# First expert's weights in quarters behind each head's copies, and rough scores and scores issued earlier

## The chip, the cores and the metric

The kernel runs on one NeuronCore of a Trainium2 chip. The metric is the device time of one execution in microseconds (us). All times below come from timed runs or from one profiled execution of the same program.

## The reference

Three stages follow each other, in float32. Attention has 2 batches, 8 heads, 576 positions and head size 64, with a causal mask and a bias from a running sum of `s`. Its output, 1152 rows of 512, goes through a sparse mixture of 8 experts (two experts a row), and then through a second mixture in which every row visits all 8 experts.

```python
scores = scale * q @ k.T                      # attention, per batch and head
scores = where(causal, -1e9, scores + minimum(-(cum_i - cum_j), 0))
attn = exp(scores - max); attn /= attn.sum(-1) + 1e-9
x = (attn @ v)                                # 1152 x 512
...
h = maximum(x[mask] @ w1[e], 0)               # sparse: the two best experts of a row
out[mask] += top2_w * (h @ w2[e])
...
out += P[:, e:e+1] * (maximum(x @ w1[e], 0) @ w2[e])   # dense: all 8 experts, P balanced in 8 steps
```

## The kernel before

Each engine runs its own written-out list of instructions, and they meet at semaphores. The change touches the attention stage and its borders only.

Attention is cut into 80 steps `k`: 8 heads, two halves (batches) a head, five tiles a half. Five steps are a unit, ten are a head. In step `k` TensorE (PE) issues, in this order: the rough scores of a later step (`rough`, L567), which exist only to find each row's maximum; transposes that turn the row maxima into a row (`turn_max`, L579), at two places in a unit; the scores of a later step (`scores`, L598 and L599); and the product of the probabilities with v (`mix`, L614). VectorE (DVE) takes each row maximum (L1041). ScalarE (ACT) puts turned maxima in place (L846), and takes the exponentials (L835 to L838). GpSimd (POOL) clears the diagonal block of the probabilities (`cut`, L479), which `mix` waits for.

How far each thing runs ahead of `mix` is set by a few numbers (L258 to L264):

```python
ROUGH_AHEAD, SCORES_AHEAD = 11, 3
WARM_UPS = 7
K_HIGH_AHEAD, Q_HIGH_AHEAD, LOW_AHEAD = 16, 15, 13
```

A head needs its inputs split into a high and a low float32r part. For head `h` ACT makes the high part of k (`high_k`, L853, starting 16 steps before the head's first mix) and of q (`high_q`, L860, one step later). SyncE's DMA queue (SP) then copies the high part of k to a second place (`double_k`, L335) and the high part of q (`double_q`, L339). POOL subtracts to make the low parts in eight pieces (`low_part`, L469), one a step, each ahead of that step's `cut`. `rough` of a head's first step waits for `double_k`'s copy, and `scores` for `double_q`'s.

In the profile most of these tiles carry the name of the storage they lie in: `w1l` holds k's top tiles, `w2h` the k tiles with the low part, `w2l` the q tiles. So `w1l<-w2h` is `double_k`, `q_two<-w2l` is `double_q`, `w2h<-k_raw` on ACT is `high_k`, `w2l<-q_raw` is `high_q`, `bank<-w1l,w2l` on PE is `rough`.

SP issues all loads of attention in one order: for head `h` the raw q and k (`load_raw`, L319 and L320), the sums, v, then `double_k(h)`, then `double_q(h)`. In head 4 it also issues the gate weights and both weight matrices of the first expert, `raw1` and `raw2`, 2 MB each, ahead of `double_k(4)` (L369, L370). ACT casts `raw1` in four pieces near the end of attention (`high_w1`, L864); POOL makes the low parts from them when all scores are done (L501).

Before the first rough scores PE runs 7 idle matmuls of 512 columns that only keep it busy (`keep_warm`, L620), and one of 256 columns in each of the 11 steps before step 0.

Of the kernel before, what the change touches and what calls it, by code (L numbers as in the profile page):

```python
# [27 lines left out]
def build(nc, qT, kT, v_rows, v_tail, s, wg, wn, noise, w1, w2, gate2, w1b, w2b, out, cum_dram, x_dram, y_dram):  # L28
    H, HD, _ = qT.shape
    B = 2  # L30
    S = qT.shape[2] // B
    G = B * H
    E, _, DC, F = w1.shape
    FC = F // P
    DM = DC * P
# [7 lines left out]
    STEPS = ST + 1  # L43
# [6 lines left out]
    with ExitStack() as ctx:  # L50
        def sb(name, shape, dt=F32, where=ctx):
            return where.enter_context(nc.sbuf_tensor(name, shape, dt))

        def sem(name):
            return ctx.enter_context(nc.semaphore(name))
# [3 lines left out]
        raw1 = sb("raw1", [P, DC, F])  # L59
        raw2 = sb("raw2", [P, FC, DM])  # L60
# [107 lines left out]
        mixed = sem("mixed")  # L168
        sums_own = sem("sums_own")
        head_done = sem("head_done")  # L170
        gates_loaded = sem("gates_loaded")
        noise_loaded = sem("noise_loaded")
        dve = sem("dve")
# [32 lines left out]
        SP_ = Stage("sparse")  # L206
# [48 lines left out]
            return n % XT_BANKS  # L255

        MAX_BANKS, MAX_AT, SCORES_AT, OUT_AT = 3, 3, 4, 6
        ROUGH_AHEAD, SCORES_AHEAD = 11, 3  # L258

        WARM_UPS = 7  # L260
        LOW_CHUNKS = 4
        LOW_COLS = N // LOW_CHUNKS
        LOWS = 2 * LOW_CHUNKS
        K_HIGH_AHEAD, Q_HIGH_AHEAD, LOW_AHEAD = 16, 15, 13  # L264

        def unit_of(k):

# [27 lines left out]

        def turns_at(k):

            first, rest = divmod(k + ROUGH_AHEAD - 3, STEPS), divmod(k + ROUGH_AHEAD - 6, STEPS)
            found = []
            if first[1] == 0 and 0 <= first[0] < G:  # L300
                found.append((first[0], 0))
            if rest[1] == 0 and 0 <= rest[0] < G:
                found.append((rest[0], 1))
            return found
# [6 lines left out]
        def _(sp):  # L311
# [4 lines left out]
            def load_raw(h):  # L316
                w = h % RAW_RING
                for half in range(2):
                    sp.dma_start(k_raw[half * HD:(half + 1) * HD, w, :], kT[h]).then_inc(k_loaded[w], 16)  # L319
                sp.dma_start(q_raw[:, w, :], qT[h]).then_inc(q_loaded[w], 16)  # L320

            def load_v(h):
                w = h % V_RING
                sp.dma_start(v_sb[:, w, 0:ST, 1:1 + P], v_rows[h]).then_inc(v_loaded[w], 16)
                sp.dma_start(v_sb[0:HALF, w, ST, 1:1 + P], v_tail[h]).then_inc(v_loaded[w], 16)

            def load_cum(h):
                w = h % HEADS_RING
                sp.dma_start(k_top[w][HD:HD + 1, :].bitcast(F32), cum_dram[h:h + 1]).then_inc(cum_loaded[w], 16)
                sp.dma_start(k_top[w][HD + 1:HD + 2, :].bitcast(F32), low_dram[h:h + 1]).then_inc(cum_loaded[w], 16)  # L330

            def double_k(h):
                w = h % HEADS_RING
                sp.wait_ge(k_high, h + 1)
                sp.dma_start(k_top[w][0:HD, :].bitcast(F32), k_two[w][0:HD, :].bitcast(F32)).then_inc(k_doubled[w], 16)  # L335

            def double_q(h):
                sp.wait_ge(q_high, h + 1)
                sp.dma_start(q_two[HD:P, h % Q_RING, :].bitcast(F32), q_top[h % HEADS_RING][0:HD, :].bitcast(F32)).then_inc(q_doubled[h % Q_RING], 16)  # L339
# [17 lines left out]
            for h in range(2, H):  # L357
                sp.wait_ge(low, LOWS * (h - 1))
                load_raw(h)
                if h >= HEADS_RING:  # L360
                    sp.wait_ge(scores_ready, HEAD * (h - HEADS_RING + 1))
                    load_cum(h)
                if h >= V_RING:
                    sp.wait_ge(mixed, HEAD * (h - V_RING + 1))
                    load_v(h)
                if h == 4:
                    for c, g in enumerate((wg, wn, gate2)):
                        sp.dma_start(gates[:, :, c * E:(c + 1) * E], g).then_inc(gates_loaded, 16)
                    sp.dma_start(raw1[:], w1[0]).then_inc(SP_.raw1_loaded, 16)  # L369
                    sp.dma_start(raw2[:], w2[0]).then_inc(SP_.raw2_loaded, 16)  # L370
                double_k(h)
                sp.wait_ge(scores_ready, HEAD * (h - Q_RING + 1))
                double_q(h)

            sp.wait_ge(head_done, G)
            sp.dma_start(noise_sb[:], noise).then_inc(noise_loaded, 16)
# [172 lines left out]
        def _(pe):  # L549

            def rough(k):
                h, b, t = head_of(k), half_of(k), rough_tile(k)
                w, rows, width = h % HEADS_RING, rows_in(t), min(S, (t + 1) * P)
                if k % HEAD == 0:
                    pe.wait_ge(q_high, h + 1)
                    if h == 0:
                        pe.wait_ge(k_first, 1)
                    else:
                        pe.wait_ge(k_doubled[w], 16 * (h // HEADS_RING + (w > 0)))
                    pe.wait_ge(cum_loaded[w], 32 * (h // HEADS_RING) + 32)  # L560
                if k >= 2:
                    pe.wait_ge(max_ready, k - 1)
                first = (0, 2, 0, 1, 2)[k % STEPS]
                q = q_top[w][0:HD + 2, b * S + t * P:b * S + t * P + rows]
                for c0 in range(0, width, BANK):
                    c1 = min(width, c0 + BANK)
                    mm = pe.matmul(bank[0:rows, first + c0 // BANK, 0:c1 - c0], q, k_top[w][0:HD + 2, b * S + c0:b * S + c1],  # L567
                                   start=True, stop=True)
                mm.then_inc(rough_ready, 1)

            def turn_max(n, part):
                tiles = TURNED[part]
                pe.wait_ge(max_ready, STEPS * n + (2 if part == 0 else STEPS))
                if n or part:
                    pe.wait_ge(max_placed, 2 * n + part)
                for t in tiles:
                    rows = rows_in(t)
                    at = (t - tiles[0]) * P
                    mm = pe.transpose(bank[0:3, MAX_AT, at:at + rows], aug[0:rows, n % MAX_RING, t, :], ident[0:rows, 0:rows])  # L579
                mm.then_inc(max_turned, 1)  # L580

            def scores(k):
                n, h, b, s_ = unit_of(k), head_of(k), half_of(k), k % STEPS
                w = h % HEADS_RING
                if k % HEAD == 0:
                    pe.wait_ge(low, LOWS * (h + 1))
                    pe.wait_ge(q_doubled[h % Q_RING], 16 * (h // Q_RING) + 16)
                if s_ == 0:
                    pe.wait_ge(max_placed, 2 * n + 2)
                if k >= 2:  # L590
                    pe.wait_ge(prob_ready, k - 1)
                pieces = ((s_, s_ * P, S if s_ else ST * P, 0),) if s_ < ST else ((0, ST * P, S, 0), (ST, ST * P, S, HALF))
                for j, i0, i1, at in pieces:
                    wide = rows_in(j)
                    c = slice(b * S + j * P, b * S + j * P + wide)
                    r_ = slice(b * S + i0, b * S + i1)
                    dst = bank[0:wide, SCORES_AT + k % 2, at:at + i1 - i0]
                    pe.matmul(dst, k_top[w][:, c], q_top[w][:, r_], start=True, stop=False)  # L598
                    mm = pe.matmul(dst, k_two[w][:, c], q_two[:, h % Q_RING, r_], start=False, stop=True)  # L599
                mm.then_inc(scores_ready, 1)  # L600
# [18 lines left out]
            def keep_warm(cols):  # L619
                pe.matmul(bank[:, BANKS - 1, 0:cols], ones[:], causal[:, 0:cols], start=True, stop=True)  # L620

            pe.wait_ge(const_ready, 6)
            for _ in range(WARM_UPS):
                keep_warm(BANK)
            for k in range(-ROUGH_AHEAD, ALL):
                if k + ROUGH_AHEAD < ALL:
                    rough(k + ROUGH_AHEAD)
                if k < 0:
                    keep_warm(BANK // 2)
                for n, part in turns_at(k):  # L630
                    turn_max(n, part)
                if 0 <= k + SCORES_AHEAD < ALL:
                    scores(k + SCORES_AHEAD)
                if k >= 0:
                    mix(k)
# [189 lines left out]
        def _(act):  # L825
# [34 lines left out]
                act.copy(q_top[h % HEADS_RING][0:HD, :], q_raw[:, w, :]).then_inc(q_high, 1)  # L860

            def high_w1(c):
                act.wait_ge(SP_.raw1_loaded, 16)
                act.copy(w1h[:, c, :], raw1[:, c, :]).then_inc(SP_.w1h_ready, 1)  # L864

            for k in range(-K_HIGH_AHEAD, ALL):
# [530 lines left out]
```

## Time and profile before

| what | value |
|---|---|
| timed runs, median of 3 | 1328.84 us (1328.59 to 1331.26) |
| the profiled execution's own time | 1328.57 us |
| its span in the profile | 1326.8 us |
| TensorE busy / weight load busy | 1273.5 us (96%) / 1127.3 us (85%) |
| VectorE / ScalarE / GpSimd busy | 37% / 27% / 11% |
| mean granted TensorE clock | 0.932 of full |

The span begins with the first instruction; the time has 1.8 us around it. The granted clock is 1.0 (2.4 GHz) or 0.5 (1.2 GHz) at any moment, and a mean between tells how the stretch is shared. Attention runs from the start to about 190 us, the routing of the rows to the experts from there to about 232 us, the sparse experts to about 500 us, and the dense ones to the end. A matmul's end is modelled, so PE busy for 100% of a stretch does not mean that its array works all the time.

### The profile page before, as it was taken

What the parts mean: (1) busy time and instruction counts of PE and PEld (TensorE: products, weight loads), DVE (VectorE), ACT (ScalarE), POOL (GpSimd) and SP (SyncE); (2) the same over time, 40 slices, a digit from 0 to 9 for tenths busy, and PEclk for the clock granted to TensorE, in tenths of its full rate; (3) what the DMA queues carried; (4) which work ended last, traced back from release to release, by engine and by line L of the source; (5) the groups of instructions that cost most, each with busy time, mean ns of one, the idle gap of its engine ahead of it and who ended that gap; (6) DMA issues with size and microseconds to landing.
All of it is one profiled execution on the core that took longest, in us unless ns stands there. A gap on an engine that the chain in (4) does not pass through costs nothing.

```text
span 1326.8 us, 17434 instructions
## 1 busy us (share of the span) xinstructions
PE 1273.5 (96%) x6613; PEld 1127.3 (85%) x6613; DVE 490.3 (37%) x1089; ACT 362.8 (27%) x680; POOL 150.8 (11%) x220
## 2 busy tenths in 40 slices
PE   8889983999999996999999999999999999999999
PEld 6768882888888885899999999999999999999998
DVE  5423334755555454144323323323323323323321
ACT  4523332444444432212212212212212212212211
POOL 7623330111111044100000000000000000000000
PEclk9955556999999997999999999999999999999999
DMA  6742022444444452301101101101101101100000
GB/s 150 226 98 63 19 70 91 155 168 169 172 174 168 176 167 78 128 1 64 64 1 64 63 0 63 63 0 63 63 0 63 63 0 63 63 0 0 24 24 24
DMA packets 23397, 102.97 MB, mean 78 GB/s; under 512 B 4416, under 2 KB 9024, under 8 KB 19264
## 3 DMA queue, kind: packets, MB, share of 16 engines
q1 hardware_dynamic: 16928, 85.97, 19.3%
q0 software_dynamic: 3360, 11.01, 2.8%
q10 hardware_dynamic: 3072, 5.51, 1.2%
q8 instruction: 22, 0.36, 0.1%
q14 instruction: 15, 0.12, 0.0%
HBM read 87.75 MB, written 10.30 MB: 74 GB/s over the span
## 4 chain that ended last, share of the span: by engine, by line
PE 93%; DVE 3%; issue 1%; DMA 1%; ACT 1%; POOL 0%; SPq 0%; POOLq 0%; DVEq 0%
PE bank L699 13%; PE bank L698 13%; PE bank L697 13%; PE bank L679 13%; PE bank L681 13%; PE bank L680 13%; PE bank L614 6%; PE bank L567 2%; PE bank L598 2%; PE bank L599 2%; PE bank L579 1%; PE bank L731 1%; DMA x_sb<-x_dram,gather_at 1%; PE bank L643 0%; PE bank L620 0%
## 5 line engine op out<-in xcount | busy, mean ns | idle before, releaser
L679 PE MATMUL bank<-xTh,w1h 128*128 128x384 f32 (+1 forms) x1024 | 343.2, 335 | 3.0 <-DVE xTl L1089 1.6
L680 PE MATMUL bank<-xTl,w1h 128*128 128x384 f32 (+1 forms) x1024 | 340.7, 333 | 0.0
L681 PE MATMUL bank<-xTh,w1l 128*128 128x384 f32 (+1 forms) x1024 | 340.7, 333 | 0.0
L907 ACT ACTIVATE hh<-bank 128x384 fp32r<-128x384 f32 (+1 forms) x256 | 123.5, 482 | 654.5 <-PE bank L681 652.6
L699 PE MATMUL bank<-w2h,hl 128*128 128x512 f32 (+1 forms) x768 | 302.2, 393 | 0.0
L698 PE MATMUL bank<-w2l,hh 128*128 128x512 f32 (+1 forms) x768 | 300.8, 392 | 0.0
L697 PE MATMUL bank<-w2h,hh 128*128 128x512 f32 (+1 forms) x768 | 299.7, 390 | 0.0
L1109 DVE SCALAR_TENSOR_TENSOR hl<-bank,hh 128x384 fp32r<-128x384 f32 (+1 forms) x256 | 139.6, 545 | 367.0 <-ACT hh L907 362.2
L679 PEld LDWEIGHTS bank<-xTh,w1h 128*128 128x128 f32 x1024 | 193.9, 189 | 5.5 <-issue 2.1
L680 PEld LDWEIGHTS bank<-xTl,w1h 128*128 128x128 f32 x1024 | 194.0, 189 | 1.2
L681 PEld LDWEIGHTS bank<-xTh,w1l 128*128 128x128 f32 x1024 | 193.7, 189 | 0.0
L698 PEld LDWEIGHTS bank<-w2l,hh 128*128 128x128 f32 (+1 forms) x768 | 141.7, 184 | 34.4
L697 PEld LDWEIGHTS bank<-w2h,hh 128*128 128x128 f32 (+1 forms) x768 | 141.6, 184 | 32.9
L699 PEld LDWEIGHTS bank<-w2h,hl 128*128 128x128 f32 (+1 forms) x768 | 141.7, 185 | 32.3
L1136 DVE SCALAR_TENSOR_TENSOR x_sb<-bank,share_now,x_sb 128x512 f32<-128x512 f32 x63 | 47.3, 750 | 259.5 <-PE bank L699 259.5
L614 PEld LDWEIGHTS bank<-v_sb,probT 128*128 128x128 f32 (+2 forms) x480 | 82.5, 251 | 9.4 <-issue 4.3
L614 PE MATMUL bank<-v_sb,probT 128*128 128x65 f32 (+2 forms) x480 | 86.4, 335 | 0.0
L1113 DVE TENSOR_TENSOR w2l<-raw,w2h 128x512 fp32r<-128x512 f32 x120 | 83.0, 692 | 0.0
L1041 DVE CUSTOM_DVE_ANT_0 unused<-bank,causal 64x576 f32<-64x576 f32 (+4 forms) x80 | 43.0, 542 | 101.9 <-PE bank L567 101.7
L911 ACT CAST w2h<-raw 128x512 fp32r<-128x512 f32 x128 | 78.3, 612 | 0.0
L1077 DVE TENSOR_TENSOR w1l<-raw,w1h 128x1024 fp32r<-128x1024 f32 x60 | 69.5, 1221 | 2.9 <-ACT w1h L886 2.9
L886 ACT CAST w1h<-raw 128x1024 fp32r<-128x1024 f32 x60 | 58.6, 1060 | 0.0
(168 smaller groups left out, 745.1 us busy)
## 6 DMA issues: line engine op xcount, KB each, us to landing
raw<-in_w SPq DMA_DIRECT2D x16, 2048.0 KB, 8.0
raw<-in_w1b SPq DMA_DIRECT2D x8, 2048.0 KB, 7.7
raw<-in_w2b SPq DMA_DIRECT2D x8, 2048.0 KB, 7.7
k_raw<-in_kT SPq DMA_DIRECT2D x16, 288.0 KB, 4.5
y_dram<-x_sb ACTq DMA_DIRECT2D x16, 256.0 KB
q_raw<-in_qT SPq DMA_DIRECT2D x8, 288.0 KB, 5.4
q_two<-w2l SPq DMA_DIRECT2D x8, 288.0 KB, 3.2
x_dram<-x_sb SPq DMA_DIRECT2D x1, 2304.0 KB, 9.3
```

Of the source, the lines that this page charges most:

```text
L614: mm = pe.matmul(bank[rows, OUT_AT + n % 2, t * (HD + 1):(t + 1) * (HD + 1)], probT[0:wide, n % UNIT_RING, at:at + nrow], v_sb[0:wide, w, ...
L679: pe.matmul(dst, w1h[:, c, fs], xTh[:, c, ts], start=(c == 0), stop=False)
L680: pe.matmul(dst, w1h[:, c, fs], xTl[:, c, ts], start=False, stop=False)
L681: mm = pe.matmul(dst, w1l[:, c, fs], xTh[:, c, ts], start=False, stop=(c == DC - 1))
L697: pe.matmul(dst, hh[:, f, ts], w2h[:, f, :], start=(f == 0), stop=False)
L698: pe.matmul(dst, hh[:, f, ts], w2l[:, f, :], start=False, stop=False)
L699: mm = pe.matmul(dst, hl[:, f, ts], w2h[:, f, :], start=False, stop=(f == FC - 1))
L907: act.activation(hh[:, f, 0:n_cols], bank[:, f % UP_BANKS, 0:n_cols], ACT.Relu).then_inc(st.hh_ready, 1)
L911: act.copy(w2h[:, f, :], raw2[:, f, :]).then_inc(st.w2h_ready, 1)
L1077: v.tensor_tensor(w1l[:, c, :], raw1[:, c, :], w1h[:, c, :].bitcast(F32), ALU.subtract).then_inc(st.w1_ready, 1)
L1109: v.scalar_tensor_tensor(out=hl[:, f, 0:n_cols], in0=bank[:, f % UP_BANKS, 0:n_cols], scalar=0.0, in1=hh[:, f, 0:n_cols].bitcast(F32), op0 ...
L1113: v.tensor_tensor(w2l[:, f, :], raw2[:, f, :], w2h[:, f, :].bitcast(F32), ALU.subtract).then_inc(st.w2_ready, 1)
```

## The change

The first expert's `raw1` is loaded in four quarters of 512 KB, one behind `double_q` of heads 3, 4, 5 and 6, each with a semaphore of its own; `raw2` goes behind the last head's `double_q`. Rough scores run 13 steps ahead where they ran 11, scores 4 where they ran 3. Row maxima are turned one step later with respect to the rough scores. `high_k` and `high_q` start two steps sooner, the low parts one. There are 9 keep-warm matmuls at the start where there were 7, and the short ones stop four steps before step 0.

```diff
+        first_w1 = [sem(f"first_w1_{c}") for c in range(DC - 1)]
...
-        ROUGH_AHEAD, SCORES_AHEAD = 11, 3
-
-        WARM_UPS = 7
+        ROUGH_AHEAD, SCORES_AHEAD = 13, 4
+
+        WARM_UPS = 9
...
-        K_HIGH_AHEAD, Q_HIGH_AHEAD, LOW_AHEAD = 16, 15, 13
+        K_HIGH_AHEAD, Q_HIGH_AHEAD, LOW_AHEAD = 18, 17, 14
...
-            first, rest = divmod(k + ROUGH_AHEAD - 3, STEPS), divmod(k + ROUGH_AHEAD - 6, STEPS)
+            first, rest = divmod(k + ROUGH_AHEAD - 4, STEPS), divmod(k + ROUGH_AHEAD - 7, STEPS)
...
                 if h == 4:
                     for c, g in enumerate((wg, wn, gate2)):
                         sp.dma_start(gates[:, :, c * E:(c + 1) * E], g).then_inc(gates_loaded, 16)
-                    sp.dma_start(raw1[:], w1[0]).then_inc(SP_.raw1_loaded, 16)
-                    sp.dma_start(raw2[:], w2[0]).then_inc(SP_.raw2_loaded, 16)
                 double_k(h)
                 sp.wait_ge(scores_ready, HEAD * (h - Q_RING + 1))
                 double_q(h)
+                if h - 3 in range(DC):
+                    sp.dma_start(raw1[:, h - 3, :], w1[0, :, h - 3]).then_inc(first_w1[h - 3] if h - 3 < DC - 1 else SP_.raw1_loaded, 16)
+            sp.dma_start(raw2[:], w2[0]).then_inc(SP_.raw2_loaded, 16)
...
-                if k < 0:
+                if k < -SCORES_AHEAD:
                     keep_warm(BANK // 2)
...
-                act.wait_ge(SP_.raw1_loaded, 16)
+                act.wait_ge(first_w1[c] if c < DC - 1 else SP_.raw1_loaded, 16)
```

Three places show what moves. On SP's queue before, from the v tail of head 4 to the raw loads of head 5 (`raw<-in_w` of 128x4096 are the two weight matrices):

```order
L325 DMA v_sb<-in_v_tail 64x128
L368 DMA gates<-in_wg 128x4x8
L368 DMA gates<-in_wn 128x4x8
L368 DMA gates<-in_gate 128x4x8
L369 DMA raw<-in_w 128x4096
L370 DMA raw<-in_w 128x4096
L335 DMA w1l<-w2h 64x1152
L339 DMA q_two<-w2l 64x1152
L319 DMA k_raw<-in_kT 64x1152 x2
```

The same place of SP's queue after the change:

```order
L326 DMA v_sb<-in_v_tail 64x128
L369 DMA gates<-in_wg 128x4x8
L369 DMA gates<-in_wn 128x4x8
L369 DMA gates<-in_gate 128x4x8
L336 DMA w1l<-w2h 64x1152
L340 DMA q_two<-w2l 64x1152
L374 DMA raw<-in_w 128x1024
L320 DMA k_raw<-in_kT 64x1152 x2
```

Nothing large is left ahead of `double_k(4)`; a quarter of 512 KB now stands between `double_q(h)` and the raw loads of head `h + 1`, for `h` from 3 to 6.

On ACT before, unit 1 of head 0 with the copies for head 2 (`w2h<-k_raw` is `high_k(2)`, `w2l<-q_raw` is `high_q(2)`, `probT<-bank` the exponentials):

```order
L835 ACTIVATE probT<-bank 128x512
L835 ACTIVATE probT<-bank 128x448
L853 CAST w2h<-k_raw 128x1152
L835 ACTIVATE probT<-bank 128x320
L860 CAST w2l<-q_raw 64x1152
L846 CAST w2l<-bank 3x384
```

On ACT after, the same unit:

```order
L837 ACTIVATE probT<-bank 128x512
L855 CAST w2h<-k_raw 128x1152
L837 ACTIVATE probT<-bank 128x448
L862 CAST w2l<-q_raw 64x1152
L837 ACTIVATE probT<-bank 128x320
L848 CAST w2l<-bank 3x384
```

Counted in exponentials the two copies stand one place sooner; counted in mixes, two steps.

On PE before, the border between start-up and step 0 (`bank<-w2l,w1l` and `bank<-q_two,w2h` are scores, `bank<-causal,ones` the keep-warm matmuls, `bank<-v_sb,probT` the first mix):

```order
L598 MATMUL bank<-w2l,w1l 128x512
L599 MATMUL bank<-q_two,w2h 128x512
L567 MATMUL bank<-w1l,w2l 128x128
L620 MATMUL bank<-causal,ones 128x256
L598 MATMUL bank<-w2l,w1l 128x448
L599 MATMUL bank<-q_two,w2h 128x448
L567 MATMUL bank<-w1l,w2l 64x512
L567 MATMUL bank<-w1l,w2l 64x64
L620 MATMUL bank<-causal,ones 128x256
```

On PE after, from the same scores:

```order
L600 MATMUL bank<-w2l,w1l 128x512
L601 MATMUL bank<-q_two,w2h 128x512
L569 MATMUL bank<-w1l,w2l 64x512
L569 MATMUL bank<-w1l,w2l 64x64
L600 MATMUL bank<-w2l,w1l 128x448
L601 MATMUL bank<-q_two,w2h 128x448
L569 MATMUL bank<-w1l,w2l 128x512
```

The rough scores of head 1 (64x512, which wait for `double_k(1)`) now follow the first scores at once, with no keep-warm matmul between.

## Rows read from the trace of the kernel before

**Rows 1.** The chain that ended last: start us, us, what.
```profile
31.65 0.47 PE bank L614 x4
...
38.40 0.47 PE bank L614 x4
...
62.22 10.44 issue
72.66 0.71 PE bank L567 x2
...
78.54 0.91 PE bank L614 x4
...
90.82 0.91 PE bank L614 x4
```
**Rows 2.** Windows of attention: busy us of each engine, then PEclk, DMA share, GB/s.
```profile
24.90:58.62 33.72, 33.72 (x267) 28.48 (x266) 17.31 (x74) 21.01 (x46) 20.89 (x44) 1.00 0.68 172
62.22:72.66 10.44, 0.00 (x1) 0.03 (x1) 0.00 (x0) 0.00 (x0) 2.44 (x5) 0.56 0.98 268
78.54:164.50 85.96, 85.96 (x373) 71.45 (x373) 26.10 (x106) 29.18 (x64) 28.65 (x60) 0.50 0.21 49
170.90:189.90 19.00, 18.98 (x95) 16.96 (x94) 2.12 (x10) 5.67 (x13) 6.73 (x13) 0.50 0.00 1
```
**Rows 3.** DMA issues between 56 and 80 us: KB each, us to landing.
```profile
w1l<-w2h SPq DMA_DIRECT2D x1, 288.0 KB, 16.3
```
**Rows 4.** Timeline of SP's queue: start us, us, engine, line, operands.
```profile
53.55 0.63 SPq L369 DMA_DIRECT2D raw<-in_w  x1
...
56.29 0.53 SPq L335 DMA_DIRECT2D w1l<-w2h  x1
```
**Rows 5.** Head 3's raw loads, issue and landing, and ACT's first copy.
```profile
32.21 1.42 SPq L319 DMA_DIRECT2D k_raw<-in_kT  x2
...
k_raw<-in_kT SPq DMA_DIRECT2D x2, 288.0 KB, 4.7
...
40.00 0.60 ACT L835 ACTIVATE probT<-bank 128x512 f32<-128x512 f32 x1 [0.35 <-PE bank L599]
41.64 1.15 ACT L853 CAST w2h<-k_raw 128x1152 fp32r<-128x1152 f32 x1
```
**Rows 6.** The page's row of 2 MB weight loads.
```profile
raw<-in_w SPq DMA_DIRECT2D x16, 2048.0 KB, 8.0
```
**Rows 7.** PE's start, and the clock there by second.
```profile
2.43 7.77 PE L620 MATMUL bank<-causal,ones 128*128 128x512 f32 x14 [2.43 <-POOL causal L442]
...
8.75 0.19 PEld L620 LDWEIGHTS bank<-causal,ones 128*128 128x128 f32 x1 [0.24 <-issue]
...
12.16 0.60 PE L567 MATMUL bank<-w1l,w2l 66*64 66x512 f32 x2 [1.97 <-DMA w1l<-x_dram]
...
12.00:13.00 1.00, 0.83 (x3) 0.68 (x4) 0.08 (x1) 0.00 (x0) 1.00 (x2) 0.65 0.79 230
```
**Rows 8.** Timeline, ACT's copy of head 2's k.
```profile
28.91 1.15 ACT L853 CAST w2h<-k_raw 128x1152 fp32r<-128x1152 f32 x1 [0.67 <-DMA k_raw<-in_kT]
```
**Rows 9.** Timeline, POOL's first low part of head 5, and PE's mix behind it.
```profile
58.77 0.79 POOL L469 TENSOR_TENSOR q_two<-q_raw,w2l 64x288 fp32r<-64x288 f32 x1 [3.19 <-PE bank L599]
59.52 0.29 POOL L479 TENSOR_SCALAR_AFFINE_SELECT probT<-probT 128x128 f32<-128x128 f32 x1
60.02 0.78 PE L614 MATMUL bank<-v_sb,probT 128*128 128x65 f32 x6
```
**Rows 10.** Timeline of the end of attention.
```profile
184.33 5.54 PE L614 MATMUL bank<-v_sb,probT 128*128 128x65 f32 x28
185.87 9.85 POOL L501 TENSOR_TENSOR w1l<-raw,w1h 128x1024 fp32r<-128x1024 f32 x4
191.23 2.02 DVE L1147 CAST gate_w<-gates 128x64 fp32r<-128x64 f32 x1
195.78 0.18 DVE L1147 CAST gate_w<-gates 128x32 fp32r<-128x32 f32 x1
```

## Prediction

> **What bounds the kernel now.** I read the page's clock line first, then the chain of waits in order of time, then windows by stage, then the DMA issues around the one hole that the chain shows. The span is 1326.8 us inside a time of 1328.57 us. PE is busy for 96% of it, so anything that shortens the kernel either removes a PE wait or makes PE's own work quicker.
>
> In attention both are to be had. The same mix of a unit returns every 6.75 us early on (31.65 to 38.40) and every 12.28 us later (78.54 to 90.82) [rows 1]. Windows show why: up to 58.62 us the granted clock is 1.00 (2.4 GHz), from 78.54 us on it is 0.50 (1.2 GHz), with PE busy all the time in both [rows 2]. So the stream is paced by PE at either clock, 12.28 / 6.75 = 1.82 times slower at the low one. Between the two lies a PE wait of 10.44 us, at whose beginning the clock is still full, and during which it falls [rows 1, 2]. It does not come back for the rest of attention.
>
> The wait is the first rough scores of head 4. They need `double_k(4)`, issued at 56.29 and landed 16.3 us later, at 72.6 [rows 3, 4]; PE starts at 72.66. Right ahead of it on SP's queue stand the two loads of 2 MB, the first issued at 53.55, the second behind it [rows 4].
>
> **The change part by part.**
>
> *The two weight loads leave the place ahead of `double_k(4)`.* The copy then lands like the undisturbed loads, in about 5 us [rows 5], where the wait leaves 5.9 us (56.29 to 62.22), and `high_k` is issued a further step sooner against the exponentials. The wait goes: 10.4 us.
>
> *The clock stays up.* For 33.7 us the same mixed stream held 1.00 with no wait in it [rows 2], and what ended that was the wait. With the wait gone I take full clock to the end of attention. Steps 29 to 68 are 40 steps, 8 units, from 72.66 to about 170.9: 8 x (12.28 - 6.75) = 44.3 us. The last 11 steps, without rough scores, took 19.0 us at 0.50 [rows 2]; at the unit's ratio 10.4 us, so 8.6 us less. What is late next there is ACT, busy 5.7 us of that stretch, so it still hides. Together 52.9 us.
>
> *The quarters.* 2 MB lands in 8.0 us [rows 6], so I take 2.0 us a quarter; the upper bound is 4.7 us, what a raw copy of 288 KB takes to land. A quarter delays the raw loads of the next head. Head 3's k was issued from 32.21 on (the second half 0.7 us later) and landed at about 37.6; ACT copied it at 41.64 [rows 5]. After the change ACT wants it one exponential sooner, at 40.6. The slack is 3.0 us, less 2.0 for the quarter: 1.0 us left, so cost 0; at the upper bound it would be 1.7 us late. `raw2` goes when nothing of attention is behind it, and is not needed for over 100 us. Cost 0.
>
> *Start-up.* The 7 warm-ups end at 10.2, PE then waits 1.97 us for the sums, and the clock falls to 0.50 as the first rough scores run [rows 7]. Each warm-up is two of the 14 instructions, and late ones come every 0.19 + 0.24 = 0.43 us, so two more warm-ups end at 11.9, before the rough scores can start at 12.16: free, and the clock should not fall there. The first steps then go at the full clock, some 0.8 us less each for three of them, a part of which waits on DVE anyway. Against that stand two more rough scores and one more scores ahead of step 0 (about 1 us), and a hole of about 0.7 us for `double_k(1)`, an estimate: its rough scores are wanted one keep-warm matmul and one scores sooner, and the copy comes some 0.5 us sooner. The first mix comes about where it did; what is issued earlier is missing at the end: two rough scores and one scores are less than the 1.35 us that a whole step takes (6.75 / 5), and I take 1.0 us less there. Bounds of start-up and this: -2 to +2 us.
>
> *Head 2's copies.* Even before, ACT waited 0.67 us for head 2's k, which landed at 28.9 [rows 8]. SP's order up to there is as it was. The change wants it about two steps sooner. Behind that wait on ACT stand the exponentials of steps 6 and 7, and behind those PE's scores of steps 8 and 9, which need their banks. With the load landing near 28.2 (SP issues it a little sooner, as its wait ahead is ACT's first copies) and a copy of 1.15 us, step 6's exponential ends near 29.9 where step 8's scores would like to start at 28.9: a PE wait of about 1.0 us, once. It cancels the 1.0 us of the last paragraph. Bounds 0 to 2 us.
>
> *POOL's low parts one step sooner.* The first low part of a head waits for scores (PE), and the `cut` is queued behind it, and the mix behind that. Before, the cut ended at 59.81 and the mix started at 60.02 [rows 9]: 0.2 us of cover. The mix that now follows comes after a block of 2 matmuls where it was 4, about 0.35 us sooner. So 0.15 to 0.2 us, in 6 heads: 1.2 us. Bounds 0 and 3.
>
> *The border behind attention.* POOL starts `w1l` when all scores are done, and while it runs for 9.85 us, DVE's copy of 128x64 takes 2.02 us where a like one after it takes 0.18 [rows 10]. At the full clock PE's last 28 matmuls take 3.1 us and not 5.5, so 2 us more of POOL's work lie behind attention's end and ahead of DVE's. I take 1.9 us; bounds 0 and 2.5 (one more of POOL's four pieces). The Trainium skill's GPSIMD Engine Reference (Specifications) says that GpSimd shares its SBUF interfaces with VectorE and that copies in a two-port mode and operations with two SBUF inputs contend; the trace's 2.02 against 0.18 us agrees, and the sum is the same without it.
>
> The rest is shifted and not changed. When the clock rises again in the routing stage can move by 2 us either way.
>
> **The sum.** 10.4 + 52.9 = 63.3 us gained; 0 for start-up with head 2, 1.2 for POOL, 1.9 at the border: 60.2 us. 1328.57 - 60.2 = 1268.4 us; the median of the runs lies 0.3 us above the profiled one, so I say 1268.5.
>
> **The rivals.**
>
> *A, the clock falls in start-up (slower).* The mixed stream never raises the clock in 117 us at 0.50 [rows 2]; once it falls it is lost until attention ends. It fell after a gap of 1.97 us at 10.2 [rows 7] and in the wait at 62.2. The changed start-up has holes of its own, 0.7 us for `double_k(1)` and 1.0 us at step 8, and its last four steps have no keep-warm matmuls. For it: both gaps come in thin streams. [...] Price: 25 steps (4 to 28) at 2.46 instead of 1.35 us, +28 us, less the wait of 10.4, less 1 at the end: about 17 us slower, 1345.
>
> *B, a quarter makes a head late.* If a quarter costs over 3 us, head 4's k misses ACT, scores follow, and the clock falls again at about the same place. Then only the long wait shrinks to 2 us or so: 1320. If it happens at a later head, each head before it saves 11.1 us: 1309, 1298, 1287. Speaking for it: DMA share 0.68 already at the full clock [rows 2]. Against: at 172 GB/s now and 512 KB more per 13.5 us it becomes 211, below the 268 of the crowded window.
>
> *C, the full clock does not last.* That it held for 34 us does not show that it holds for 100. The Trainium skill, TensorE: Matmul & The Clock Gate (A second HAM failure mode: psum-queue depth-cycling), tells of a kernel in which short idles between groups of matmuls make the clock go up and down. As a mechanism here: half of the remaining stream at each clock gives 10.4 + 26 us less 3, 1295. The trace speaks against it, with five units in a row at 6.75 us.
>
> **Chances.** Forecast 0.80, its own range 1261 to 1277 (the bounds above, which do not all fall on one side). A 0.10, B 0.07, C 0.03. About 0.2% (2.7 us) is what a measurement of this kernel can tell from no change; only the slack between A and B falls there. Faster 0.88, same 0.02, slower 0.10. For the 8 in 10 I reach from 1260 to 1287, up to the mildest form of B.
>
> **What would show it.** The page's clock line at 9 without a 5 through the slices of attention; a unit every 6.75 us to the end; attention over at about 128 us where it was 190; no PE wait above 1.5 us between the first mix and the last; `w1l<-w2h` landing in 3 to 6 us for head 4; ACT waiting for `k_raw` in head 2, and not in heads 4 to 7; two to three DVE operations of 2 us behind attention's end. A clock of 0.5 anywhere between 15 and 125 us makes the forecast wrong.

## The result, and the profile after

The changed kernel runs at 0.9539 of the time before (95% interval 0.9512 to 0.9567): 1267.45 and 1267.89 us against a median of 1328.71. The profiled execution took 1267.45 us with a span of 1265.7. One thing must be said to read the numbers: the changed kernel has two kinds of execution, one at 1267 to 1270 us and one at 1341 to 1352 us, and the ratios here compare the first kind alone.

The first four executions took 1267.45, 1348.51, 1267.89 and 1341.14 us; of all 17 that were timed, nine were of the first kind and eight of the second. Their mean is 1304.6 us, so on the average the change as it stands gives 24 us, and not the 61 of its first kind. The kernel before has no such pair (1325 to 1332 us in all 41 executions). The second kind is rival A of the prediction, and most of the experiments are about it.

From the profile's page of the changed kernel, the span, the busy line and the clock line; the latter's digits are the granted clock in tenths, one for each fortieth of the span:

```profile
span 1265.7 us, 17437 instructions
PE 1220.8 (96%) x6613; PEld 1082.7 (86%) x6613; DVE 491.4 (39%) x1089; ACT 361.0 (29%) x680; POOL 150.1 (12%) x220
PEclk9999679999999979999999999999999999999999
```

Before, slices 3 to 6 (the rest of attention) read 5555. Now the first four are at 9, and the 6 and 7 behind them are the routing stage, which had its stretches at half clock before as well.

Windows of the changed kernel; columns: stretch, length, then busy time and count of PE, PE's weight loads, DVE, ACT and POOL, then granted clock, DMA share, GB/s:

```profile
12.19:23.57 11.38, 10.36 (x57) 7.61 (x58) 7.19 (x27) 5.25 (x9) 8.78 (x13) 1.00 1.00 231
23.80:122.00 98.20, 97.75 (x764) 83.15 (x764) 49.32 (x204) 58.21 (x133) 58.77 (x127) 1.00 0.61 150
122.00:126.80 4.80, 4.80 (x47) 4.29 (x46) 0.96 (x5) 1.26 (x5) 3.16 (x7) 1.00 0.01 2
```

Full clock through all of attention, PE idle for only 0.45 us of 98. Attention is over at 126.8 us, where before the last mixes of [rows 10] ended at 189.9: 63.1 us sooner. The span is 61.1 us shorter, so 2.0 us are given back behind attention.

PE's waits of the changed kernel from 11 to 125 us (engine, line, what was waited for, sum, times, longest), then the DMA issues from 45 to 56 us (tile, queue, KB, us from issue to landing):

```profile
PE bank L569 <- DMA w1l<-w2h: 1.0, 1, 1.0
PE bank L600 <- ACT probT L837: 0.4, 1, 0.4
```

```profile
k_raw<-in_kT SPq DMA_DIRECT2D x2, 288.0 KB, 6.4
raw<-in_w SPq DMA_DIRECT2D x1, 512.0 KB, 6.4
...
q_raw<-in_qT SPq DMA_DIRECT2D x1, 288.0 KB, 7.7
w1l<-w2h SPq DMA_DIRECT2D x1, 288.0 KB, 3.1
```

The wait of 10.44 us [rows 1] is gone: `double_k(4)` lands in 3.1 us and not in 16.3 [rows 3]. A quarter lands in 6.4 us, and the next head's loads behind it take 6.4 us (k) and 7.7 us (q), where before the change they took 4.7 [rows 5] and 5.4. PE does not wait for them: its two waits that are left both lie ahead of 30 us. ACT does, once behind a quarter. The slowest load of k in this execution took 8.2 us to land, and ACT's copy of head 7's k waited 1.50 us for its load (the row of k's landings, then ACT's timeline):

```profile
DMA to landing us min/median/max: 3.6/5.3/8.2
...
95.66 1.15 ACT L855 CAST w2h<-k_raw 128x1152 fp32r<-128x1152 f32 x1 [1.50 <-DMA k_raw<-in_kT]
```

The chain of waits of the changed kernel in attention (start, length, what): the same mix, one unit apart each time:

```profile
39.26 0.39 PE bank L616 x4
...
45.93 0.61 PE bank L616 x4
...
52.82 0.39 PE bank L616 x4
```

The distance between mixes of one kind alternates between 6.67 and 6.89 us, where at full clock before every unit took 6.75 [rows 1]. A head has two units, so once a head something comes late. The timeline shows what: POOL makes the head's first low part from 44.80 to 45.59 us and the `cut` behind it, and PE's weight load for the mix waits 0.39 us for that `cut`:

```profile
45.54 0.29 POOL L481 TENSOR_SCALAR_AFFINE_SELECT probT<-probT 128x128 f32<-128x128 f32 x1
45.88 0.52 PEld L616 LDWEIGHTS bank<-v_sb,probT 128*128 128x128 f32 x4 [0.39 <-POOL probT L481]
```

DVE's timeline behind attention, changed kernel (start, length, line, operation, tiles; in brackets the idle time before it), then POOL's:

```profile
128.15 1.76 DVE L1149 CAST gate_w<-gates 128x64 fp32r<-128x64 f32 x1
...
130.20 2.19 DVE L1152 TENSOR_TENSOR fold<-ident 32x16 f32<-32x16 f32 x1
132.43 0.18 DVE L1149 CAST gate_w<-gates 128x32 fp32r<-128x32 f32 x1
132.64 2.25 DVE L1150 TENSOR_TENSOR gate_w<-gates,gate_w 128x32 fp32r<-128x32 f32 x1
...
135.12 3.21 DVE L1084 TENSOR_TENSOR xTl<-bank,xTh 128x512 fp32r<-128x512 f32 x5
```

```profile
125.02 9.83 POOL L503 TENSOR_TENSOR w1l<-raw,w1h 128x1024 fp32r<-128x1024 f32 x4
```

Three small DVE operations now take about 2 us, while a like one between them takes 0.18. POOL's four instructions are 9.83 / 4 = 2.46 us each if they are equally long, so they end at 127.48, 129.94, 132.39 and 134.85, and the three held operations at 129.91, 132.39 and 134.89: each ends with one of POOL's. POOL's work ends 8.05 us behind the last mix, where it ended 5.8 us behind it before [rows 10].

### The profile page after: what moved, and what is told of

It reads as the page before. It is cut to its first block, busy times and chain, and to the rows that moved or that the text cites. A ratio compares the mean times of both kernels' runs of the same rounds, so it can differ in the third digit from the quotient of the medians.

```text
span 1265.7 us, 17437 instructions
## 1 busy us (share of the span) xinstructions
PE 1220.8 (96%) x6613; PEld 1082.7 (86%) x6613; DVE 491.4 (39%) x1089; ACT 361.0 (29%) x680; POOL 150.1 (12%) x220
## 4 chain that ended last, share of the span: by engine, by line
PE 93%; DVE 3%; DMA 2%; ACT 1%; issue 1%; POOL 1%; SPq 0%; POOLq 0%; DVEq 0%
PE bank L701 14%; PE bank L700 14%; PE bank L699 14%; PE bank L681 13%; PE bank L683 13%; PE bank L682 13%; PE bank L616 4%; PE bank L569 1%; PE bank L600 1%; PE bank L601 1%; PE bank L622 1%; PE bank L733 1%; DMA x_sb<-x_dram,gather_at 1%; PE bank L581 1%; PE bank L645 0%
## 5 line engine op out<-in xcount | busy, mean ns | idle before, releaser
L616 PEld LDWEIGHTS bank<-v_sb,probT 128*128 128x128 f32 (+2 forms) x480 | 54.5, 173 | 6.4 <-POOL probT L481 2.4
L616 PE MATMUL bank<-v_sb,probT 128*128 128x65 f32 (+2 forms) x480 | 59.1, 257 | 0.0
```

Of the source, the lines that this page charges most:

```text
L616: mm = pe.matmul(bank[rows, OUT_AT + n % 2, t * (HD + 1):(t + 1) * (HD + 1)], probT[0:wide, n % UNIT_RING, at:at + nrow], v_sb[0:wide, w, ...
```

## The experiments

All times are of the device, in us. Three chips were used for these runs, and on each the kernel before ran beside the others: its median was 1328.89 beside runs 1 to 4, 1328.78 beside runs 5, 7, 8 and 9, and 1328.49 beside runs 6, 10, 11 and 12. On the first of these chips 4 of 7 executions of the changed kernel were of the second kind, on the third 2 of 6; on the second, that of runs 5, 7, 8 and 9, the changed kernel was not run. `keep_warm(n)` is a matmul whose result nobody reads.

**1. The changed kernel again**, unchanged, for its two kinds.

> The changed kernel once more, to count its executions. So far two took 1267.45 and 1267.89 us and two 1341.14 and 1348.51. Theory H (holes in start-up): the two PE waits that the change opened, 0.95 us at 20.1 for head 1's k and about 0.8 us at 28.4 behind ACT's wait for head 2's k, sometimes make the clock fall, and it then stays at 0.5 to the end of attention. H expects two kinds of execution and nothing between them: 1266 to 1269 us, and 1340 to 1350 us. Rival R (the clock falls anywhere in the 100 us of mixed stream at full clock): times spread over the whole way between 1268 and 1345, since each head before the fall saves 11 us.

Measured: 1266.87, 1267.81, 1267.83, and 1341.56, 1345.83, 1346.48, 1348.09; ratio of the first kind 0.9534 (0.9514 to 0.9554). The profiled execution was one of the second kind, so the traces of both can be laid beside each other. Page, PE's waits from 11 to 60 us, windows, and PE's and ACT's timeline of this execution:

```profile
span 1339.8 us, 17437 instructions
PEclk9555556799999998999999999999999999999999
```

```profile
PE bank L600 <- ACT probT L837: 1.0, 1, 1.0
PE bank L569 <- issue: 0.6, 1, 0.6
```

```profile
23.00:29.00 6.00, 6.00 (x46) 5.10 (x45) 3.29 (x12) 2.64 (x9) 4.55 (x10) 1.00 0.86 216
...
31.00:32.00 1.00, 1.00 (x12) 0.86 (x12) 0.00 (x0) 0.98 (x3) 0.00 (x0) 1.00 0.83 175
32.00:33.00 1.00, 1.00 (x8) 1.00 (x9) 0.70 (x5) 0.93 (x4) 0.32 (x1) 0.65 0.58 120
...
34.00:200.00 166.00, 166.00 (x733) 142.89 (x733) 46.30 (x190) 55.16 (x123) 57.56 (x124) 0.50 0.31 81
```

```profile
21.70 0.45 PE L569 MATMUL bank<-w1l,w2l 66*64 66x512 f32 x2 [0.58 <-issue]
30.58 0.36 PE L600 MATMUL bank<-w2l,w1l 67*128 67x192 f32 x1 [1.00 <-ACT probT L837]
28.93 1.15 ACT L855 CAST w2h<-k_raw 128x1152 fp32r<-128x1152 f32 x1 [2.63 <-DMA k_raw<-in_kT]
```

The clock is full up to 32 us, falls soon after the second of the two holes that the prediction named (0.58 us for head 1's rough scores, 1.00 us behind ACT's copy of head 2's k), and stays at 0.50 to the end of attention with PE busy all the time. That is rival A, place and mechanism. In the execution of the first kind the holes were these:

```profile
21.07 0.44 PE L569 MATMUL bank<-w1l,w2l 66*64 66x512 f32 x2 [0.95 <-DMA w1l<-w2h]
29.18 0.36 PE L600 MATMUL bank<-w2l,w1l 67*128 67x192 f32 x1 [0.42 <-ACT probT L837]
27.53 1.15 ACT L855 CAST w2h<-k_raw 128x1152 fp32r<-128x1152 f32 x1 [1.88 <-DMA k_raw<-in_kT]
```

**2. The loads alone**: the kernel before with the quarters, nothing else of the change.

```
 ROUGH_AHEAD, SCORES_AHEAD = 11, 3        # as before; WARM_UPS = 7
-    sp.dma_start(raw1[:], w1[0]) ...     # both, ahead of double_k(4)
-    sp.dma_start(raw2[:], w2[0]) ...
+    sp.dma_start(raw1[:, h - 3, :], w1[0, :, h - 3]) ...   # behind each head's copies
+sp.dma_start(raw2[:], w2[0]) ...         # behind the heads
```

> Only the quarters (and raw2 behind the last head); all the distances, the turning of the maxima and the warm-ups as before. H: start-up is that of the kernel before, whose executions are all within 1327 to 1331 us, so the clock is up from 15.7 us on in every one of them, and with the wait of 10.4 us gone it stays: every execution at 1266 to 1271 us, none above 1300. R: the stream at full clock is as long as in the changed kernel, so about half of the executions are slow. If the earlier issue was needed for the gain (rival S), the fast time would be well above 1270.

Measured: 1271.07 (1268.38 to 1272.69), ratio 0.9556 (0.9540 to 0.9572), no execution of the second kind. Its clock line reads

```profile
PEclk9999679999999979999999999999999999999999
```

and its units, by the chain of waits, are all 6.75 us long:

```profile
24.10 0.47 PE bank L616 x4
30.85 0.47 PE bank L616 x4
```

So 58 of the 61 us are the loads. Five executions alone do not rule the second kind out here; run 9, with the same order, adds five more without it.

**3. The order alone**: the change's distances, turns and warm-ups with the two whole loads ahead of `double_k(4)`.

```
+    sp.dma_start(raw1[:], w1[0]) ...     # both, ahead of double_k(4), as before
+    sp.dma_start(raw2[:], w2[0]) ...
-    sp.dma_start(raw1[:, h - 3, :], w1[0, :, h - 3]) ...
```

> Only the distances, the turning and the warm-ups of the change; raw1 and raw2 whole and ahead of double_k(4) as before. Both theories: the wait for double_k(4) stays (7 to 10 us), the clock falls in it, and the fast executions take 1324 to 1331 us, same as before. H: some executions are slower by another 25 us or so (clock down from start-up on), near 1355.

Measured: median of the first kind 1330.4, ratio 1.0013 (1.0000 to 1.0026), and 4 of 10 executions at 1352 to 1355. By itself the order gains nothing. The wait for `double_k(4)` is now 12.61 us in the chain of waits, 2.2 longer than [rows 1] shows: PE comes to it 1.4 us sooner and goes on 0.8 later.

```profile
60.20 0.61 PE bank L615 x4
60.81 12.61 issue
73.42 0.71 PE bank L568 x2
```

The second kind comes with the order, with or without the quarters. This kernel's profiled execution is of the first kind, and its holes in start-up were nearly those of run 1's:

```profile
21.14 0.45 PE L568 MATMUL bank<-w1l,w2l 66*64 66x512 f32 x2 [0.56 <-issue]
29.89 0.36 PE L599 MATMUL bank<-w2l,w1l 67*128 67x192 f32 x1 [0.88 <-ACT probT L836]
```

0.56 and 0.88 us and the clock stayed up; 0.58 and 1.00 and it fell.

**4 to 7. The holes filled.** Run 4 fills both with matmuls nobody reads, runs 5 and 6 the first alone (the same kernel, on two chips), run 7 the second alone.

```
+if k + ROUGH_AHEAD == HEAD:      # runs 4, 5, 6: ahead of head 1's first rough scores
+    keep_warm(BANK // 2)
+    keep_warm(BANK // 2)
 ...
+if k == STEPS - 1:               # runs 4, 7: in step 4, behind the rough scores
+    keep_warm(BANK // 2)
```

> The changed kernel with three keep-warm matmuls of 256 columns (0.43 us each at full clock) put into the two holes: two ahead of head 1's first rough scores, one in step 4 ahead of the scores that wait for ACT. H: the holes shrink to about 0.1 and 0.3 us of idle, the clock never falls, every execution at 1265 to 1270 us. R: nothing changes, half of the executions slow. If the filled matmuls are late for what they hide in, the fast time is up to 0.5 us longer.

> The changed kernel with only the first of the two start-up holes filled: two keep-warm matmuls ahead of head 1's first rough scores. In the profiled slow execution of the changed kernel the clock fell at about 32.3 us, after the second hole (1.0 us of wait for ACT's exponential, 29.6 to 30.6). Theory H2 (the second hole alone decides): still two kinds of execution, some at 1340 to 1349 us. Theory H1 (the first hole, or both together, decide): every execution at 1266 to 1271 us.

> Only the first hole filled, as before, which gave five fast executions of five (1268.3 to 1271.2). The second hole is still there, 0.5 us of wait in its profile. If the two holes together are needed for a fall (H12), all executions are fast again. If the second alone suffices (H2), some of them are at 1340 to 1349 us.

> The changed kernel with only the second hole filled: one keep-warm matmul in step 4 ahead of the scores that wait for ACT. H2: every execution at 1266 to 1271 us, none above 1300. H1: still about half of them at 1340 to 1349 us.

Measured, median and ratio: both 1269.76, 0.9552 (0.9538 to 0.9566), no PE wait of 0.2 us or more between 11 and 60 us; first alone 1269.55 and 1270.15, 0.9557 (0.9544 to 0.9570) and 0.9555 (0.9540 to 0.9570), with the second hole still there (0.5 and 0.4 us); second alone 1270.75, 0.9563 (0.9550 to 0.9576), with the first hole still at 1.0 us. None of these 20 executions was of the second kind. If every execution had the changed kernel's chance of 8 in 17, twenty without one would come in 3 of a million cases, the ten with the first hole alone filled in 1 of 600, and the five of run 7 in 1 of 24. The 8 in 17 is itself only a sample, so these odds are rough: with that taken in, ten come by chance in about 1 of 90 cases.

Run 7 did not close the second hole but made it shorter. In its profiled execution ACT waited 2.37 us for head 2's k, half a microsecond longer than in the first profile, and 0.44 us were left of the hole:

```profile
29.69 0.35 PE L600 MATMUL bank<-w2l,w1l 67*128 67x192 f32 x1 [0.44 <-ACT probT L839]
```

So it is likely that the second hole at its usual size is not enough without the first. A matmul in the first hole can also make the second one shorter, and each run has one profile, so the runs do not tell this from a second hole that decides alone where it is long.

**8. The cause of the second hole taken away**: head 2's raw loads issued two copies sooner.

```
+sp.wait_ge(low, LOWS); load_raw(2)    # ahead of double_q(1) and load_v(2)
 for h in range(2, H):
-    load_raw(h)
+    if h > 2: load_raw(h)
```

> The changed kernel with head 2's raw k and q issued ahead of double_q(1) and head 2's v, 2.3 us sooner on SP's queue; nothing is filled. This takes away what the second hole comes from (ACT's wait for head 2's k, 1.9 us in the fast profile, 2.6 us in the slow one). H2: ACT waits for less than 0.5 us, PE has no wait in steps 3 to 6, and every execution is at 1265 to 1269 us. If the clock falls for another reason (R or H1), about half remain at 1340 to 1349 us.

Measured: 1269.81 (1268.21 to 1270.21), 0.9557 (0.9544 to 0.9570), none of the second kind. ACT no longer waits for head 2's k, and PE's only wait from 11 to 60 us is head 1's first rough scores:

```profile
PE bank L572 <- issue: 0.6, 1, 0.6
```

With run 7 that makes ten executions with the second hole gone or shortened and the first still there, all of the first kind, as many as with the first hole filled. All ten ran on the chip on which the changed kernel was not run.

**9. Nine warm-ups on the kernel of run 2**, to see what start-up's clock is worth.

```
-WARM_UPS = 7
+WARM_UPS = 9
```

> The quarters alone (distances of the kernel before) with 9 warm-ups. With 7 the clock is down from about 12.3 to 15.7 us in every execution; with 9 it should stay up, and start-up gets up to 1 us shorter: 1267 to 1271 us against the 1271.1 us median with 7, all executions fast. If start-up is paced by the loads of the first heads and not by PE, no difference from 1271.

Measured: 1269.45 (1268.74 to 1271.31), 0.9555 (0.9542 to 0.9568): 1.6 us less than run 2, with ranges that overlap. The nine executions of the first kind of the changed kernel have a median of 1267.89, the ten of runs 2 and 9 together 1269.7. So executions of the first kind are about 2 us shorter with the order. In the profiles this does not come from attention: PE's last mix ends at 125.97 us in run 2 and at 126.01 in run 9, and at 126.80 in the changed kernel. From 178 to 250 us, behind the routing, the granted clock is 0.98 in runs 2 and 9 and 1.00 in the changed kernel; no run separates this from chance. Against the 2 us stand 8/17 of 77 us, some 36, which the second kind costs on the average.

**10. The changed kernel a third time**, beside the last three.

> The changed kernel once more, beside the others of this call, since the calls so far need not have had the same chip. H expects again two kinds of execution, 1266 to 1269 us and 1340 to 1350 us, some of each (so far 5 and 6). If all its executions here are fast, the five fast ones of the kernels with one hole filled say little.

Measured: 1267.93, 1268.84, 1269.41, 1269.76, and 1341.06, 1351.54; ratio of the first kind 0.9553 (0.9539 to 0.9567). The profiled one, of the first kind, had holes of 0.5 and 0.2 us, although its first rough scores started at 12.93 us and head 2's k was issued at 23.03, both later than in the profiled execution of run 1 that lost the clock. ACT waited 1.85 us for that k, not 2.63.

**11. The second hole made longer**: the three loads of the gates moved ahead of head 2's raw loads.

```
+for c, g in enumerate((wg, wn, gate2)):        # ahead of load_raw(2)
+    sp.dma_start(gates[:, :, c * E:(c + 1) * E], g).then_inc(gates_loaded, 16)
-    if h == 4: (the same three)
```

> The changed kernel with the three small gate loads ahead of head 2's raw loads on SP's queue instead of in head 4. They take 1.9 us of issue, so head 2's k lands about 2 us later and PE's second hole grows from about 0.5 to 1.0 us to 2.3 to 3 us. H (length of the hole decides): the clock falls in every execution, about 1343 to 1351 us, none near 1268. If the length does not matter, about half are fast, at 1269 to 1271.

Measured: 1342.96, 1344.84, 1345.71, 1349.40, all four of the second kind; ratio 1.0139 (1.0121 to 1.0157). PE's waits from 11 to 60 us, and windows around the hole:

```profile
PE bank L599 <- ACT probT L836: 2.9, 1, 2.9
PE bank L568 <- issue: 0.5, 1, 0.5
```

```profile
29.00:30.00 1.00, 0.00 (x0) 0.00 (x0) 0.03 (x2) 0.00 (x0) 0.00 (x0) 1.00 0.16 37
30.00:31.00 1.00, 0.00 (x0) 0.00 (x0) 0.00 (x0) 0.97 (x1) 0.00 (x0) 0.83 0.01 5
31.00:32.00 1.00, 0.32 (x1) 0.32 (x2) 0.00 (x0) 1.00 (x3) 0.00 (x0) 0.50 0.00 0
```

Here the clock falls inside the hole. The same place with 2.9 us for 0.2 to 1.0 turns half of the executions into all of them, and the price is the same.

**12. A better kernel**: the changed one with the second hole's cause gone (run 8), the first hole filled (run 5), and the six DVE operations on the gates' weights moved from behind attention into its last steps, ahead of POOL's `w1l`.

```
 for k in ...:                       # DVE's steps of attention
+    if k == ALL - 2 * STEPS + 2:
+        split_gates()               # the six operations of lines 1149 to 1152
```

> A version meant to be the best: the changed kernel with head 2's raw loads sooner, the first hole filled, and the six DVE operations on the gate weights moved from behind attention into it, where DVE idles (step 72). Behind attention three of them were held up for about 2 us each while POOL made w1l, and the first subtraction for the transposed x came only at 135.1 us, 8.3 us after PE's last mix. If that subtraction reads PSUM and one SBUF tile and is not held up by POOL, it starts at about 2.7 us after the last mix, and up to 5 us are gained: 1262 to 1266 us, all fast. If POOL holds it up too, at most 1 us: 1267 to 1269.

Measured: 1261.47 (1260.63 to 1261.68), ratio 0.9496 (0.9483 to 0.9508), all five of one kind, no PE wait from 11 to 60 us. Against those of the first kind in run 10 (median 1269.1) it is 7.7 us less, more than the 5 us that were expected at most. DVE's timeline of this kernel:

```profile
119.17 0.20 DVE L1078 CAST gate_w<-gates 128x64 fp32r<-128x64 f32 x1
119.40 0.23 DVE L1079 TENSOR_TENSOR gate_w<-gates,gate_w 128x64 fp32r<-128x64 f32 x1
119.66 0.17 DVE L1081 TENSOR_TENSOR fold<-ident 32x16 f32<-32x16 f32 x1
...
129.63 1.47 DVE L1102 TENSOR_TENSOR xTl<-bank,xTh 128x512 fp32r<-128x512 f32 x2 [1.90 <-ACT xTh L898]
131.26 2.48 DVE L1102 TENSOR_TENSOR xTl<-bank,xTh 128x512 fp32r<-128x512 f32 x4 [0.16 <-ACT xTh L898]
```

The three that took 2 us take 0.2, and `xTl` starts 5.5 us sooner (129.63 for 135.12). Attention itself ends at 126.41 us, 0.4 us sooner than in the first profile. Which of the three parts gives how much of the 7.7 us was not measured.

## Why the prediction was right, and where it was not

The forecast of 1268.5 us was met by 1267.45 and 1267.89, and for its reasons, in nine executions of 17; the other eight lie where rival A was put, and the clock of 0.50 from 34 us on in run 1's profile is the prediction's own sign of being wrong. With eight in 17 of the second kind, two of each among the first four is no surprise, and the chance of 0.80 for the forecast was too high.

*The wait* (10.4 us) went as worked out, and *the clock* (52.9 us) stayed up to the end of attention, by the loads alone (run 2). Predicted end of attention about 128 us, measured 126.8.

*The quarters* were priced at 2.0 us on the next head's loads, within a slack of 3.0, with 4.7 as the bound. They cost 1.7 (6.4 against 4.7) for head 4, 2.6 for head 7 (7.3), and up to 3.5 for one load of k (8.2). The sign "ACT waiting for `k_raw` in head 2, and not in heads 4 to 7" did not hold: ACT waited 1.50 us in head 7, and 0.46 in the profile of run 10. Cost 0 for PE was right all the same, and not for the slack of 1.0 us that was worked out: that was used up, and behind ACT's copy there was room enough that PE never waited. So it was partly luck, as the condition of rival B ("over 3 us") was met for one load. Rival B did not come in any of the 61 executions with quarters: none lies between 1273 and 1340 us.

*Start-up* came out nearly as drawn: in the first profile the two extra warm-ups are free (the rough scores start at 12.19 us, 12.16 before) and the clock stays up at 12 us. In the profiles of runs 1 and 10 the rough scores stood behind the warm-ups until 12.81 and 12.93, so there they cost some 0.7 us. Of the holes, the one for `double_k(1)` is 0.95 us for an estimated 0.7 (0.5 and 0.6 in other executions), and head 2's is 0.42 for 1.0 (1.00 and 0.2 in others).

*POOL's low parts* (1.2 us) were put too high. The 0.15 to 0.2 us show in each head's longer unit, 6.89 for 6.75; but the other unit is shorter, 6.67, so that the mean of 6.78 costs 0.03 us a unit, some 0.4 us in all.

*The border* was put at 1.9 us with two to three DVE operations held; three are, POOL ends 2.2 us later behind attention than before, and 2.0 us are given back there. What I had not seen is how much more lay there: the six operations out of POOL's way, with the two repairs of start-up, give 7.7 us (run 12).

What failed is the weight given to *rival A*, the chance of 0.10. Its mechanism, place and price were right (1345 for 1341 to 1352). It named both holes, 0.7 and 1.0 us, and knew of two waits after which the clock fell, of 1.97 us [rows 7] and 10.44 us [rows 1]. That those two were longer does not show that shorter ones are harmless. In run 1 the clock fell behind a hole of 1.00 us, 8 us after one of 0.58, and the second kind came in 8 of 17 executions. None of the 25 executions with one or both holes filled, shortened or removed (runs 4 to 8) lost the clock. That makes it likely that the two holes act together, where the prediction has a size for each and nothing on the pair; it is not shown (see runs 4 to 8).

Rival C, a full clock that does not last, is out: none of the 40 executions of runs 2, 4 to 9 and 12 lost it.

**What stays open.** Why one execution of the same program has its clock fall and another not. Each size is from one profiled execution: 0.95 and 0.42, 0.54 and 0.19, 0.56 and 0.88, and run 7's 0.97 and 0.44 kept the clock; 0.58 and 1.00, and 0.5 and 2.9, lost it. So the second hole was the longer one wherever the clock fell, but 0.88 and 1.00 lie too close to call this shown. A late start-up as such does not decide: run 10's profiled execution was as late as that of run 1 and kept the clock. Whether the length of the second hole decides, the sum of both, or something that these profiles do not show, no run here tells.

## What to carry to other kernels

Look for a large load that is issued ahead of a small copy on the same queue: 4 MB ahead of 288 KB cost 10.4 us as a wait and some 53 as a clock that did not come back; half of it in quarters, each behind a head's own copies, made PE wait for nothing. An order that issues further ahead must be checked at its start, where it makes holes: fill them with matmuls that nobody reads, which cost 1 to 2 us here (runs 4 and 6 against the first kind on the same chip), since holes of 0.6 and 1.0 us cost 77 us when the clock falls. For this kernel the loads alone (run 2, 1271.07) are safer than the whole change, whose mean is 1304.6. And time such a change in many executions: the changed kernel showed its second kind in 8 of 17, and four executions need not show both.

## What the runs showed of the hardware

- At half clock (0.50) the same stream of matmuls ran with PE busy for 166.0 of 166.0 us and the granted clock did not rise; at full clock it ran for 98 us with PE busy for 97.75 and it did not fall (the two kinds of execution of the changed kernel).
- One program on one core had two outcomes, 6% apart. The profiled execution of the slower had two PE waits ahead of the fall, 0.58 and 1.00 us; with 2.9 us in the place of the second the slower came in four of four (run 11).
- DVE operations that read SBUF alone and began while a POOL instruction ran lasted until about its end (1.76, 2.19 and 2.25 us for 0.2), but the subtraction with one input in PSUM and one in SBUF ran beside the same POOL work at 2.48 / 4 = 0.62 us, its length elsewhere 0.69 (run 12).
